# The first expert's second weight split on VectorE alone, and new places for the work around it

## The reference, cut to what matters

```python
x = attn(x, state)                    # 8 * (512 + 32) = 4352 rows
x = max(0.01 * (x @ w_in), x @ w_in) @ w_out
e_idx = argmax(x @ w_gate)
gate_w = softmax(x @ w_gate)[e_idx]
eom = sigmoid(x @ w_output_gate)
for e in range(8):
    m = e_idx == e
    out[m] = gate_w[m] * eom[m, e] * (relu(x[m] @ w1[e]) @ w2[e])
```

## Time and profile before

| | |
|---|---|
| median of 3 runs | 1198.63 us (1198.11 to 1200.19) |
| the profiled execution | 1198.8 us, with a span of 1197.0 us |
| PE busy | 1155.9 us (97% of the span) |
| DVE busy | 564.4 us (47%) |
| ACT busy | 400.3 us (33%) |
| POOL busy | 160.1 us (13%) |
| mean granted TensorE clock | 0.993 of full speed |

### The profile page before, as it was taken

How to read it: one execution, slowest core, us unless ns; L and a number is a source line. 1 busy time by engine, 2 the same in 40 slices (tenths; PEclk the granted TensorE clock), 3 DMA queues, 4 the chain that set the end, 5 groups by cost and what they waited for, 6 DMA issues and landing times.

```text
span 1197.0 us, 18214 instructions
## 1 busy us (share of the span) xinstructions
PE 1155.9 (97%) x6706; PEld 948.7 (79%) x6707; DVE 564.4 (47%) x1246; ACT 400.3 (33%) x751; POOL 160.1 (13%) x200
## 2 busy tenths in 40 slices
PE   5999999999999999999999997999999999999995
PEld 3777778777787777787777887899998989888884
DVE  5574474563654744745634446352232225255221
ACT  4443433333424434333333333141221124244211
POOL 1000001010010010010100104331212213133221
PEclk9999999999999999999999998999999999999998
DMA  9211111110120211110100400561111111533110
GB/s 353 105 40 36 36 41 36 36 41 36 41 71 1 76 36 36 40 36 1 36 1 26 154 36 27 166 224 44 53 35 53 46 42 51 187 121 107 44 43 29
DMA packets 37726, 78.44 MB, mean 66 GB/s; under 512 B 9095, under 2 KB 9351, under 8 KB 37640
## 3 DMA queue, kind: packets, MB, share of 16 engines
q1 hardware_dynamic: 28549, 52.92, 12.6%
q0 software_dynamic: 9120, 24.76, 6.5%
HBM read 59.75 MB, written 20.61 MB: 67 GB/s over the span
## 4 chain that ended last, share of the span: by engine, by line
PE 79%; DVE 14%; ACT 4%; issue 1%; DMA 0%; POOL 0%; SPq 0%; DVEq 0%; ACTq 0%; POOLq 0%
PE bank L470 23%; PE bank L472 22%; PE bank L471 22%; PE bank L521 2%; PE bank L585 2%; DVE gT_lo L1071 2%; PE bank L490 2%; ACT gT_hi L894 2%; DVE g_buf L1067 2%; PE bank L725 1%; PE bank L531 1%; DVE a_buf L1042 1%; DVE a_buf L1032 1%; ACT a2T L841 1%; DVE small L1031 1%
## 5 line engine op out<-in xcount | busy, mean ns | idle before, releaser
L470 PE MATMUL bank<-wout_lo,gT_hi 128*128 128x512 f32 x544 | 219.0, 403 | 0.0
L472 PE MATMUL bank<-wout_hi,gT_hi 128*128 128x512 f32 x544 | 212.7, 391 | 0.0
L471 PE MATMUL bank<-wout_hi,gT_lo 128*128 128x512 f32 x544 | 212.0, 390 | 0.0
L1067 DVE TENSOR_TENSOR g_buf<-g_buf,bank 128x512 f32<-128x512 f32 (+1 forms) x144 | 94.4, 655 | 116.1 <-ACT g_buf L888 116.0
L470 PE MATMUL bank<-xgT_lo,w_hi 128*128 128x256 f32 x512 | 146.1, 285 | 2.6 <-DVE xgT_lo L1267 1.0
L471 PE MATMUL bank<-xgT_hi,w_lo 128*128 128x256 f32 x512 | 145.7, 285 | 0.0
L472 PE MATMUL bank<-xgT_hi,w_hi 128*128 128x256 f32 x512 | 145.6, 284 | 0.0
L888 ACT ACTIVATE g_buf<-bank 128x512 f32<-128x512 f32 (+1 forms) x144 | 82.9, 575 | 171.6 <-PE bank L472 147.5
L1071 DVE TENSOR_TENSOR gT_lo<-g_buf,gT_hi 128x512 fp32r<-128x512 f32 (+1 forms) x144 | 95.6, 664 | 91.4 <-ACT gT_hi L894 90.8
L965 ACT ACTIVATE hT_hi<-bank 128x256 fp32r<-128x256 f32 x128 | 49.0, 384 | 239.8 <-PE bank L472 228.2
L894 ACT CAST gT_hi<-g_buf 128x512 fp32r<-128x512 f32 (+1 forms) x144 | 85.9, 597 | 116.8 <-DVE g_buf L1067 116.7
(11 more groups left out here) (199 smaller groups left out, 1696.2 us busy)
## 6 DMA issues: line engine op xcount, KB each, us to landing
raw<-w_dram SPq DMA_DIRECT2D x20, 1024.0 KB
rows_dram<-y_buf SPq DMA_DIRECT2D x8, 1032.0 KB
XT<-xT_in_dram SPq DMA_DIRECT2D x8, 1024.0 KB, 5.4
X<-x_in_dram SPq DMA_DIRECT2D x8, 1024.0 KB, 5.4
win<-w_in_dram SPq DMA_DIRECT2D x4, 1024.0 KB, 13.3
y_buf<-w_out_dram POOLq DMA_DIRECT2D x6, 512.0 KB, 7.1
stT<-stT_in_dram SPq DMA_DIRECT2D x8, 128.0 KB, 2.2
yT<-w_out_dram POOLq DMA_DIRECT2D x2, 512.0 KB, 7.9
```

The lines of the kernel that those rows point to most:

```text
L470: pe.matmul(o, l_hi, r_lo, start=first, stop=False)
L471: pe.matmul(o, l_lo, r_hi, start=False, stop=False)
L472: return pe.matmul(o, l_hi, r_hi, start=False, stop=last)
L1067: dve.tensor_tensor(g_buf[:, n, 0:w], g_buf[:, n, 0:w], up_b[n][:, 0:w], ALU.max).then_inc(g_ready, 1)
```

## The change

Four things are changed, all in the first expert step:
- POOL no longer subtracts for pieces 4 to 7. DVE does it, one piece ahead of the state logits' copy, and one each behind `route_slots` and the `h_lo` pairs of f = 2, 3 and 4, 5.
- PE runs `state_logits()` ahead of group f = 1 in place of ahead of f = 0, the rank matmuls ahead of f = 4 in place of f = 2, and the turning of the second batch inside the output product, ahead of f = 5 of u = 1.
- ACT's four casts are interleaved with the hidden layer's casts.
- DVE works out the whole plan behind the last `h_lo`, and makes the second batch's `xgT_lo` between the two halves' outputs.

```diff
@@ gpsimd
             set_slots(B, 4)
-            pool.wait_ge(e_lo_done, DC)
-            for i in range(DC, 8):
-                pool.wait_ge(e_hi_done, i + 1)
-                r, hi, lo = expert_parts(0, i)
-                pool.tensor_tensor(lo, r, hi.bitcast(fp32), ALU.subtract).then_inc(e_lo_done, 1)
             set_slots(B + 1, 2)
@@ tensor
                 flip_y(B, 1)
-                state_logits()
                 pe.wait_ge(xg_lo_done, 2)
                 pe.wait_ge(e_lo_done, DC)
                 for f in range(F2):
-                    if f == 2:
+                    if f == 1:
+                        state_logits()
+                    elif f == 2:
+                        pe.wait_ge(lg_copied, B + 1)
+                    elif f == 4:
                         ranks(B, 2, rank_bank=oacc[0])
-                        pe.wait_ge(lg_copied, B + 1)
                     if f >= 4:
                         pe.wait_ge(h_lo_done, f - 3)
...
+                        if u == 1 and f == 5:
+                            flip_rows(1)
                         last = product(oacc[u][:, :], hT_hi[:, f, us], hT_lo[:, f, us], w2_hi[0][:, f, :], w2_lo[0][:, f, :],
                                        f == 0, f == F2 - 1)
                     last.then_inc(o_ready, 1)
-                flip_rows(1)
@@ scalar
-            split_expert(0, 0, (4, 5, 6, 7))
+            split_expert(0, 0, (4,))
+            hidden_T(0, (0,))
+            split_expert(0, 0, (5,))
             exp_gates(B, 2)
-            hidden_T(0)
+            hidden_T(0, (1, 2))
+            split_expert(0, 0, (6,))
+            hidden_T(0, (3, 4))
+            split_expert(0, 0, (7,))
+            hidden_T(0, (5, 6, 7))
             rows_hi(1)
@@ vector
             rows_lo(0)
+            split_expert(0, 0, (4,))
             copy_state_logits()
             route(B, 2)
+            h_lo(0, 0)
             route_gate(B, 2)
-            h_lo(0, 0)
             h_lo(0, 1)
             route_ranks(B, 2, rank_bank=oacc[0])
             route_slots(B, 2, state=True)
+            split_expert(0, 0, (5,))
             h_lo(0, 2)
             h_lo(0, 3)
-            plan_order()
+            split_expert(0, 0, (6,))
             h_lo(0, 4)
             h_lo(0, 5)
-            plan_steps()
+            split_expert(0, 0, (7,))
             h_lo(0, 6)
             h_lo(0, 7)
+            plan_order()
+            plan_steps()
             dve.wait_ge(slots_in, 16)
...
-            for u in range(2):
-                dve.wait_ge(o_ready, u + 1)
-                last = dve.tensor_scalar(o_buf[:, u, :], oacc[u][:, :], s_now[:, u:u + 1], None, ALU.mult)
-            last.then_inc(o_kept, 3)
+            dve.wait_ge(o_ready, 1)
+            dve.tensor_scalar(o_buf[:, 0, :], oacc[0][:, :], s_now[:, 0:1], None, ALU.mult)
             rows_lo(1)
+            dve.wait_ge(o_ready, 2)
+            dve.tensor_scalar(o_buf[:, 1, :], oacc[1][:, :], s_now[:, 1:2], None, ALU.mult).then_inc(o_kept, 3)
```

More of the change, by code:

```diff
@@ L960, in rows_hi, with hidden_T @@
                     act.copy(xgT_hi[:, 2 * n:2 * n + 2, :], t_b[n][:, :].rearrange("p (c t) -> p c t", c=2)).then_inc(xg_hi_done, 1)
-            def hidden_T(i):
-                for f in range(F2):
+            def hidden_T(i, steps=range(F2)):
+                for f in steps:
                     act.wait_ge(h_ready, F2 * i + f + 1)
```

## The result

The kernel after the change takes 1195.43 us (median of 10 runs, 1194.05 to 1197.72). The kernel before took 1198.62 (median of 10). The ratio is 0.9972, with a 95% interval from 0.9964 to 0.9981, so the change is worth 3.2 us, or 0.28%. I predicted 1196.9 with a range of 1194.0 to 1199.0. The time lies in the range, and next to the rival in which PE keeps its full clock (1195.3).

What follows compares the result with a forecast made beforehand. The prediction took PE to bound the kernel, through its waits and slow stretches. A next step 3.4 us earlier, less 1.7 for the clock, gained 1.7 us: 1197.1, or 1196.9 us as a median, range 1194.0 to 1199.0.

Steps and rivals of the forecast that it cites:

- The stretch was POOL's doing: DVE beside POOL's subtractions: four instructions 6.8 us too long because of POOL; the rival denying this had chance 0.03.
- The steps up to the gather: First expert step: ranks at 739.45, pos_i done 742.05, slot_row done 752.7, both gathers landed 759.7.
- wait at the turning: PE at flip_rows(1) inside the output product: asks at 755.5 and waits 4.2 us for the gather.
- The gain at a full clock: End of the first expert step: PE starts the next step at 762.8, 3.4 us earlier than before.
- The register loads: PE's loads between the last product and next step: put at nothing, at most the earlier gap of 0.97 us.
- The clock's term: PE's new wait for the gather: the clock falls and slow matmuls cost 1.7 us.
- the two bounds: Clock in the new wait: full after a 3.72 us wait, fallen in one of 5.77; cost 0 or about 1.7.
- the first rival: New wait: the gather binds and PE keeps its full clock; 3.4 us gained, 1195.3 us; chance 0.32.
- faster: Whole kernel: faster by over 0.2% (2.4 us), below 1196.2 us; chance 0.45.
- the same: Whole kernel: within 0.2%, between 1196.2 and 1201.0 us; chance 0.49.
- the forecast case: The gather binds and the clock falls in the new wait: 1.7 us gained, 1196.9 us; chance 0.46.
- The third rival: Slot scatters beside pieces 5 and 6: DVE and POOL hold each other up; at worst 1198.9 us; chance 0.12.

Runs made afterwards that it cites:

- Run 3: Kernel after the change with the subtractions of pieces 4 to 7 back on POOL, all new places kept; 1200.88 us, ratio 1.0016 to the kernel before.
- run 9: Run 8 with five POOL copies of 128x1024 from SBUF to SBUF added from the first turning on; 1192.09 us, one execution.
- run 5: Kernel after the change with twelve unread 512-column matmuls on PE ahead of the second batch's turning; 1194.03 us, ratio 0.9957 to the kernel before.
- run 2: Kernel after the change with only the second batch's turning put back behind the output product; 1197.73 us, ratio 0.9988 to the kernel before.
- run 1: Kernel after the change measured and profiled again, no edit; 1195.62 us, ratio 0.9971 to the kernel before.
- run 8: Run 7 with slot_row ahead of piece 7 and the last two h_lo, turning ahead of f = 7; 1190.17 us, ratio 0.9929 to the kernel before.
- run 4: Kernel before with only the four subtractions moved from POOL to DVE; 1193.82 us, ratio 0.9963.
- run 7: Run 4 with the turning ahead of f = 6 of u = 1 and xgT_lo between the two outputs; 1191.99 us, ratio 0.9943 to the kernel before.
- run 10: Run 8 with five POOL fills of 128x1024 added from the first turning on; 1190.44 us, one execution.

## Why the prediction was right in range, and which term was off

**The stretch was POOL's doing: right.** Route's instructions take 0.17 to 0.19, where four in the kernel before were 6.8 us too long. Run 3 brings the stretch back with POOL's subtractions alone, and run 9 with other POOL work.

**The steps up to the gather: right.** Relative to the first turning, forecast and measured: ranks +10.2 and +10.2; end of `pos_i` +12.8 and +12.75; wait at f = 6 1.2 and 0.86; end of `slot_row` +23.4 and +22.9; landing of both gathers +30.4 and +29.9; wait at the turning 4.2 and 3.65. The slot table's load was issued at +17.7, where my sum had +17.1, and never bound: the earlier trace rows shows only the issue, not the 2.2 us of my sum, but the profile's list of transfers has 2.2 us to the landing before and 2.1 here. So it landed 2.9 us ahead of the plan's end. The half microsecond by which `slot_row` came early lies in the three pieces and six `h_lo`: 5.45 us from the end of `pos_i` to the plan (743.26 to 748.71) where I had summed 6.0.

**The gain at a full clock: right, in part by luck.** 3.4 forecast, 3.5 by run 5. My 3.1 us from the landing to the next step were the turning and nine matmuls. The register loads, which I had at nothing, take nearly the same: 3.12 us in run 2, where no product matmul lies behind the turning.

**The clock's term: mis-sized, and this is the error.** The prediction took "1.7, because the fall itself was seen after less idle time than I forecast". The fall came, as forecast, but two profiles show 1.9 and 0.9 us. The medians gained 3.2. The profile of run 1, which lies at the median, divides such a gain: 2.6 in the step and 0.8 outside it, ahead of it and behind it. So of the 1.5 us between the forecast's gain of 1.7 and the 3.2 measured, about 0.8 is the clock's price in the wait, and the rest came from outside the step, where the shorter waits for `hT_lo` lie. That rest I can't attribute to any part of the change. The mean clocks of whole executions don't help: run 8 took 1190.08 us once at 0.991 and once at 0.996. Three of the 21 executions of the kernel after took 1194.05 to 1194.17, like those of run 5. Perhaps the clock stayed full in them; none of them was profiled.

One of the two bounds was misread as well. The prediction says that a wait of 3.72 us (the `a_buf` row) "left the clock full". The clock's column says so, the matmuls behind that wait do not:

```profile
22.50 0.63 PE L471 MATMUL bank<-aT_hi,v_lo 128*128 128x512 f32 x1
22.93 0.63 PE L472 MATMUL bank<-aT_hi,v_hi 128*128 128x512 f32 x1
...
22.00:23.00 1.00, 1.00 (x3) 0.81 (x4) 0.90 (x5) 1.00 (x2) 0.00 (x0) 1.00 1.06 412
```

They follow each other at 0.43 us, the pace of the half clock (763.05 to 763.48 in the kernel after), under a granted clock of 1.00. In the kernel after the same matmuls have the same pace, and there the column shows 0.50. So that wait is no evidence for a full clock in the new one, and the first rival, with its chance of 0.32, had no other. The reader is to check the clock by the pace of the matmuls.

The error in size was to take a price seen once, after a longer wait, as fixed. The middle of my own two bounds, 0.85, would have given 3.4 - 0.85 = 2.55 and 1196.1, nearer, and would have put "faster" ahead of "the same", though with a lower bound that doesn't stand. With 1.7 us (0.14%) the forecast case was "the same"; measured is 0.28%, with an interval from 0.19% to 0.36% that only touches my bound of 0.2%.

**The register loads: the wrong bound.** "I put them at nothing ... and at most at that 0.97". Under the slow clock of the two profiles the nine matmuls do cover them; at a full clock (run 5) PE stands still for about 0.3 us behind the ninth. And the bound is false: where nothing covers them, the next step starts 3.12 us behind the landing in place of 2.00 (run 2). It did little harm here, and it spoiled my expectation of run 2.

**The third rival: real in kind, in the other direction.** The scatters and the pieces did meet. The scatters took 1.12 and 1.49 us where the kernel before had 1.00 and 0.97 (at 747.74 and 749.04), and the pieces 1.22 each, as always. It was POOL that was longer and not DVE, and the 0.64 us was covered. POOL's copy of two elements behind them took 0.97 us beside piece 7 (at 747.04), where it had 0.20 before. By the rule of the Trainium skill that I cited (SBUF — State Buffer, section "SBUF: two separate sides") I had worked out 1 to 2 us on the gather's path; the trace shows none of it on DVE. Whether a scatter counts as an instruction that reads SBUF for this purpose stays open: the rows show that it was longer, not why.

**What I didn't see.** I priced the change as one piece. Moving the subtractions is worth more alone (1193.8) than with the rest (1195.4 to 1195.6). The ranks' later place lengthens the one chain that binds once the stretch is gone, by 1.9 us up to `pos_i` (run 4). The turning in the product saves nothing on that chain; it gives some time back because the clock stays up (run 7 against run 4). My own numbers had it: I put the ranks at 739.45, where PE had been standing ready for them from 737.05 before, and I forecast a new wait of 4.2 us for the gather. I didn't ask which of the parts pulled the other way.

## What to carry to other kernels

Where small VectorE instructions lie on the path, look at what GpSimd does beside them: one long elementwise GpSimd instruction can hold a 0.2 us instruction for 2 us. When a stall is taken away, follow the same chain to what is late next, and put that chain (here `slot_row` and the gather) ahead of bulk work before moving anything else. Count what an engine's queue does behind a wait, register loads too, and treat a clock drop seen once as a spread and not as a price. Check the profile's clock against the pace of equal matmuls before you lean on it.

## What the runs showed of the hardware that I had not expected

- The price of a clock drop varies between executions of one kernel: with waits of 3.65 and 3.56 us the clock was at half for 6.9 and 3.5 us, from 2.0 us behind the last matmul's end in one and from 4.6 us behind it in the other, where PE was at work again. Idle gaps of 1.71 and 2.03 us with eight matmuls of 128 columns between them (run 2) also ended in a fall, and 1.66 and 0.68 (run 7) did not.
- The granted clock of a stretch can read 1.00 while the matmuls in it have the pace of the half clock: 0.43 us from one 512-column matmul to the next at 22.50 in the profile of before, and 0.23 at full pace.
- Twelve useless matmuls in a wait made the program 1.4 us faster (run 5).
- POOL's fills held single DVE instructions with one SBUF input by up to 0.5 us (run 10), and none with two by more than 0.1; the next step came 0.43 us later.
- Three register loads on PE's queue take 2.3 us to their end behind a wait (759.3 to about 761.6 in run 2), and delay the first matmul behind them by 1.1 us beyond the data. In seven runs (2, 4, 5 and 7 to 10) the next step starts 3.1 to 3.4 us behind the landing of the gathers, wherever the turning stands.
